# Up projection of a routed expert layer: stationary operand changed from activations to weights, with the loop unrolled by two and its addresses made in fours

## The reference

```python
def _moe2_ref(x, w_gate, w_local, w1, w2):      # x (4, 576, 512), w1 (8, 512, 1024), w2 (8, 1024, 512)
    ...
            prev_e = e
            ls = logits[b, s] - logits[b, s].max()
            p = np.exp(ls)
            p /= p.sum() + 1e-09
            h = np.maximum(x[b, s] @ w1[e], 0.0)
            out[b, s] = p[e] * (h @ w2[e])
```

## Time and profile before

| | |
|---|---|
| time, median of three runs | 987.25 us (985.24 to 988.3) |
| time of the profiled execution | 985.19 us |
| its span (first to last recorded instruction) | 983.4 us |
| PE busy | 923.3 us, 94% of the span |
| share of PE in the chain that ended last | 85% |
| experts' part of the span | from about 673 us to the end |

### The profile page before, as it was taken

How to read it: one execution, slowest core, us unless ns; L and a number is a source line. 1 busy time by engine, 2 the same in 40 slices (tenths; PEclk the granted TensorE clock), 3 DMA queues, 4 the chain that set the end, 5 groups by cost and what they waited for, 6 DMA issues and landing times.

```text
span 983.4 us, 20128 instructions
## 1 busy us (share of the span) xinstructions
PE 923.3 (94%) x7739; PEld 584.8 (59%) x7740; DVE 457.1 (46%) x843; ACT 357.5 (36%) x475; POOL 284.2 (29%) x298
## 2 busy tenths in 40 slices
PE   5899998999999999999999999928999999999996
PEld 3566666456676767677767677614555555555552
DVE  4788887464523333333333343758973773000000
ACT  3677776353211212122121112012444444444442
POOL 2467766400111102020201000002443444333331
PEclk9999999899999999999999999968999999999998
DMA  8245542525201010110101102514763672111100
GB/s 284 82 149 160 165 141 64 162 84 160 65 23 44 22 43 29 35 43 21 43 21 43 43 0 74 171 36 122 252 202 124 220 223 80 43 42 49 50 13 1
DMA packets 55340, 89.21 MB, mean 91 GB/s; under 512 B 7140, under 2 KB 26035, under 8 KB 55165
## 3 DMA queue, kind: packets, MB, share of 16 engines
q1 hardware_dynamic: 49853, 72.56, 23.7%
q0 software_dynamic: 5440, 16.00, 5.3%
HBM read 71.19 MB, written 16.55 MB: 89 GB/s over the span
## 4 chain that ended last, share of the span: by engine, by line
PE 85%; DVE 8%; DMA 3%; issue 2%; ACT 1%; SPq 1%; POOL 0%; DVEq 0%; POOLq 0%; ACTq 0%
PE psum L803 19%; PE psum L820 19%; PE psum L979 13%; PE psum L955 13%; PE psum L598 4%; PE psum L742 3%; PE psum L754 2%; PE psum L968 2%; DVE m_mem L1251 2%; DVE arena L1279 2%; PE psum L943 1%; PE psum L764 1%; PE psum L619 1%; PE psum L653 1%; PE psum L672 1%
## 5 line engine op out<-in xcount | busy, mean ns | idle before, releaser
L803 PE MATMUL psum<-m_mem,arena 128*128 (+1 forms) x1728 | 198.8, 273 | 0.3 <-DVE arena L1511 0.3
L820 PE MATMUL psum<-arena,m_mem 128*128 128x512 f16 x864 | 195.3, 379 | 0.0
L803 PEld LDWEIGHTS psum<-m_mem,arena 128*128 128x128 f16 x1728 | 168.4, 98 | 26.0 <-DVE arena L1511 0.6
L820 PEld LDWEIGHTS psum<-arena,m_mem 128*128 128x128 f16 x864 | 84.6, 98 | 90.4
L955 PE MATMUL psum<-arena,m_mem 128*128 x600 | 135.2, 382 | 0.5 <-ACT m_mem L1184 0.5
L1119 ACT ACTIVATE m_mem<-psum 128x512 f16<-128x512 f32 x72 | 43.0, 597 | 250.1 <-PE psum L803 249.1
L979 PE MATMUL psum<-arena,m_mem 128*128 x600 | 133.6, 379 | 0.0
L955 PEld LDWEIGHTS psum<-arena,m_mem 128*128 128x128 f16 x600 | 58.2, 99 | 66.6 <-issue 2.8
L1419 DVE SCALAR_TENSOR_TENSOR m_mem<-psum,m_mem 128x512 f16<-128x512 f32 x72 | 49.7, 691 | 103.4 <-ACT m_mem L1119 102.6
L979 PEld LDWEIGHTS psum<-arena,m_mem 128*128 128x128 f16 x600 | 57.7, 98 | 65.4 <-issue 0.4
L1756 POOL TENSOR_TENSOR arena<-m_mem,arena 128x1024 f16<-128x1024 f32 x9 | 18.0, 1995 | 272.2 <-ACT arena L1134 227.2
(11 more groups left out here) (220 smaller groups left out, 1156.4 us busy)
## 6 DMA issues: line engine op xcount, KB each, us to landing
dimdft_sb<-in_exp_w SPq DMA_DIRECT2D x74, 256.0 KB, 3.2
wstage<-in_exp_w SPq DMA_DIRECT2D x54, 256.0 KB, 3.2
m_mem<-in_qk SPq DMA_DIRECT2D x16, 576.0 KB, 4.5
arena<-in_v SPq DMA_DIRECT2D x32, 160.0 KB, 4.3
x_rows<-m_mem SPq DMA_DIRECT2D x16, 320.0 KB, 3.3
x_rows<-arena SPq DMA_DIRECT2D x9, 512.0 KB, 2.8
wstage<-in_mlp_w SPq DMA_DIRECT2D x16, 256.0 KB, 3.2
arena<-in_mlp_w SPq DMA_DIRECT2D x16, 256.0 KB, 2.9
```

What stands on the lines that cost most here:

```text
L803: last = nc.tensor.matmul(psum[:, 2 + k % 4, (f % 2) * 2 * P:(f % 2 + 1) * 2 * P], w1_sb[:, sp_, c, f * P:(f + 1) * P], unT[:, bass.ds(t % ...
L820: last = nc.tensor.matmul(psum[:, 6 + q, :], hT[:, k % 4, sp_, at:at + P], w2_sb[:, mp, f, :], start=f == 0 and sp_ == 0 and mp == 0, stop ...
```

## The change

`up` now takes the weights as the stationary operand and streams the activations past them. One matmul has 128x128 weights and 128 columns of tokens, so there are 8 x 4 x 3 = 96 of 128 columns in place of 24 of 512. The result is already features by tokens: `transpose_he`, `copy_heT`, `he_parts` and their semaphores go, and so do the 11 unused matmuls ahead of the last `down`. ACT's rectified parts go straight to `heT`, which now has two copies (`k % 2`), so the PE loop is unrolled by two (`turn`). `up` has a new wait for `hs_done` (banks 2 and 3 read by ACT), and `relu` new waits for `he_lo` and `blocks_done`.

```diff
+            def point(slot, places, base):
+
+                regs = [pe.alloc_register(f"weights_at{next(pointers)}") for _ in places]
+                for reg, at in zip(regs, places):
+                    pe.reg_add(reg, slot, 2 * at + base)
...
+            def pointed(at, n):
+                return slot_bytes[:, bass.ds(at, 2 * n)].bitcast(F16)
+
+            def up(k, e, slot, first):
 
                 pe.wait_ge(xeT_copied, k + 1)
                 pe.wait_ge(w_split, e * ECH + (WCH + ECH))
-                for half in range(2):
+                if not first:
+                    pe.wait_ge(hs_done, k)
+                for f in range(FE // P):
                     for c in range(DC):
-                        for sp_, mp in THREE:
-                            at = mp * EW + c * FE + half * 512
-                            last = nc.tensor.matmul(psum[:, 2 + half, :], xeT[:, sp_, c, :],
-                                                    slots[:, bass.ds(slot, 1), at:at + 512]
-                                                    .rearrange("p o n -> p (o n)"),
-                                                    start=c == 0 and sp_ == 0 and mp == 0,
-                                                    stop=c == DC - 1 and sp_ == 1)
+                        if c % 2 == 0:
+                            regs = point(slot, [wp * EW + (c + i) * FE + f * P for i in range(2) for wp in range(2)],
+                                         ARENA_AT + 2 * P - 2)
+                        for wp, mp in THREE:
+                            last = nc.tensor.matmul(psum[:, 2 + f // 4, f % 4 * P:(f % 4 + 1) * P],
+                                                    pointed(regs[wp * EW + c * FE + f * P], P), xeT[:, mp, c, :],
+                                                    start=c == 0 and wp == 0 and mp == 0,
+                                                    stop=c == DC - 1 and wp == 1)
                 last.then_inc(eh_ready, 1)
 
-            def transpose_he(k):
-
+            def down(k, turn, slot, first=False):
                 pe.wait_ge(he_lo, k + 1)
-                for i in range(2):
-                    into = psum[:, 4 + i, :].bitcast(F16)
-                    for f in range(FE // P):
-                        last = nc.tensor.transpose(into[:, f * P:(f + 1) * P], he_parts[:, i, f * P:(f + 1) * P],
-                                                   identb_sb[:, :])
-                last.then_inc(heT_ready, 1)
...
-            def experts(k, first=False, last=False, second=False):
+            def experts(k, turn, first=False, last=False, second=False):
                 e, slot = expert_of(k)
                 if not first:
                     _, last_slot = expert_of(k - 1)
-                    transpose_he(k - 1)
-                up(k, e, slot)
+                up(k, e, slot, first)
                 if not last:
                     transpose_xe(k + 1)
                 if not first:
-                    down(k - 1, last_slot, second)
+                    down(k - 1, 1 - turn, last_slot, second)
...
-            with pe.Fori(2, NBLK - 1) as k:
-                experts(k)
-            experts(NBLK - 1, last=True)
+            with pe.Fori(2, NBLK - 1, 2) as k:
+                for turn in range(2):
+                    experts(k + turn, turn)
+            experts(NBLK - 1, 0, last=True)
             _, slot = expert_of(NBLK - 1)
-            transpose_he(NBLK - 1)
-            keep_clock(2, 11)
-            down(NBLK - 1, slot)
+            down(NBLK - 1, 0, slot)
...
-            def relu(k):
+            def relu(k, first, early):
 
                 act.wait_ge(eh_ready, k + 1)
-                nc.scalar.activation(he_parts[:, 0].rearrange("p (b n) -> p b n", b=2), psum[:, 2:4, :], ACT.Relu,
+                if not first:
+                    act.wait_ge(he_lo, k)
+                if not early:
+                    act.wait_ge(blocks_done, k)
+                nc.scalar.activation(heT[:, bass.ds(k % 2, 1), 0].rearrange("p o f s -> p (o f s)"),
+                                     psum[:, 2:4, :].rearrange("p b n -> p (b n)"), ACT.Relu,
                                      scale=1.0 / WS).then_inc(he_hi, 1)
```

More of the change, by code:

```diff
@@ L21 @@
+import itertools
 import math
@@ L122, in fused_kernel @@
         x_tail = SLOT_STEP + SLOT_WORDS
+        slot_bytes = arena[:, :].bitcast(mybir.dt.uint8)
         def slot_of(e):
             return (e * 3 + 1) % NSLOT
+        ARENA_AT = 16512
         ident_sb = sb("ident_sb", [P, P], F32)
@@ L293, in fused_kernel @@
         hs = carve([FE], F32)
-        he_parts = carve([2, FE], F16)
-        heT = carve([2, FE // P, P], F16)
+        heT = carve([2, 2, FE // P, P], F16)
         xe_parts = carve([2, D], F16)
@@ L436, in fused_kernel @@
         hs_done = sem("hs_done")
-        heT_ready = sem("heT_ready")
         he_hi = sem("he_hi")
         he_lo = sem("he_lo")
-        heT_copied = sem("heT_copied")
         blocks_done = sem("blocks_done")
@@ L945, in transpose_xe @@
                 last.then_inc(xeT_ready, 1)
-            def up(k, e, slot):
+            pointers = itertools.count()
+            def point(slot, places, base):
+                regs = [pe.alloc_register(f"weights_at{next(pointers)}") for _ in places]
+                for reg, at in zip(regs, places):
+                    pe.reg_add(reg, slot, 2 * at + base)
+                return {at: pe.snap(reg, donate=True, min_val=base, max_val=base + 2 * (NSLOT * SLOT_STEP - D),
+                                    guaranteed_mod_val=0, out_of_modulus=2) - base
+                        for reg, at in zip(regs, places)}
@@ L972, in down @@
-            def down(k, slot, first=False):
-                pe.wait_ge(heT_copied, k + 1)
                 if not first:
@@ L976, in down @@
                 for f in range(FE // P):
+                    if f % 2 == 0:
+                        regs = point(slot, [mp * EW + DC * FE + (f + i) * D for i in range(2) for mp in range(2)],
+                                     ARENA_AT)
                     for sp_, mp in THREE:
[L978 to L981, removed]
+                        last = nc.tensor.matmul(psum[:, 6, :], heT[:, turn, sp_, f, :],
+                                                pointed(regs[mp * EW + DC * FE + f * D], D),
                                                 start=f == 0 and sp_ == 0 and mp == 0,
@@ L987, in expert_of @@
                 e = pe.value_load(blkexp[0:1, bass.ds(k, 1)], min_val=0, max_val=E - 1)
-                return e, pe.snap(slot_of(e))
-            def experts(k, first=False, last=False, second=False):
+                return e, pe.snap(slot_of(e) * (2 * SLOT_STEP))
+            def experts(k, turn, first=False, last=False, second=False):
                 e, slot = expert_of(k)
@@ L1004, in _ @@
             slots_second()
-            experts(0, first=True)
-            experts(1, second=True)
-            with pe.Fori(2, NBLK - 1) as k:
-                experts(k)
-            experts(NBLK - 1, last=True)
+            assert NBLK % 2 == 1
+            experts(0, 0, first=True)
+            experts(1, 1, second=True)
+            with pe.Fori(2, NBLK - 1, 2) as k:
+                for turn in range(2):
+                    experts(k + turn, turn)
+            experts(NBLK - 1, 0, last=True)
             _, slot = expert_of(NBLK - 1)
-            transpose_he(NBLK - 1)
-            keep_clock(2, 11)
-            down(NBLK - 1, slot)
+            down(NBLK - 1, 0, slot)
         @block.scalar
@@ L1185, in copy_xeT @@
                     .then_inc(xeT_copied, 1)
-            def relu(k):
+            def relu(k, first, early):
                 act.wait_ge(eh_ready, k + 1)
-                nc.scalar.activation(he_parts[:, 0].rearrange("p (b n) -> p b n", b=2), psum[:, 2:4, :], ACT.Relu,
+                if not first:
[4 more added lines that the diff above has]
+                                     psum[:, 2:4, :].rearrange("p b n -> p (b n)"), ACT.Relu,
                                      scale=1.0 / WS).then_inc(he_hi, 1)
-                nc.scalar.activation(hs.rearrange("p (b n) -> p b n", b=2), psum[:, 2:4, :], ACT.Relu, scale=1.0 / WS)\
+                nc.scalar.activation(hs, psum[:, 2:4, :].rearrange("p b n -> p (b n)"), ACT.Relu, scale=1.0 / WS)\
                     .then_inc(hs_done, 1)
[L1195 to L1200, removed]
             def weigh(k, first):
@@ L1211, in experts @@
             def experts(k, first=False, second=False, last=False):
-                if not first:
-                    copy_heT(k - 1)
-                relu(k)
+                relu(k, first, first or second)
                 if not last:
@@ L1225, in _ @@
             experts(NBLK - 1, last=True)
-            copy_heT(NBLK - 1)
             weigh(NBLK - 1, False)
@@ L1787, in he_lo_of @@
                 pool.wait_ge(hs_done, k + 1)
-                nc.gpsimd.tensor_tensor(he_parts[:, 1], hs, he_parts[:, 0], ALU.subtract).then_inc(he_lo, 1)
```

(2 more changed lines are left out.)

## The result

The changed kernel takes 970.25 us (median of four runs, 968.86 to 970.97) against 986.38 us of the kernel before, measured beside it (median of four, 985.24 to 988.3). The ratio is 0.9833, 95% interval 0.9813 to 0.9853: 1.7% faster, by 16.1 us. The forecast was 966.5, the range 962 to 979. The profiled execution took 969.82 us, its span is 968.0.

The account below looks back on a forecast made before the run. The prediction took PE's array as the bound in a steady block. Gains of 1.3 (start), 16.1 (23 blocks) and 2.0 (end), 19.4 us off 985.19, gave 965.8; it forecast 966.5 us, adjusted toward the median, range 962 to 979.

Parts of the forecast that it names:

- PE's array as the bound, and the gain per block: Steady block: array time decides; `transpose_he` saves 0.89 us, `up` at 5.37 costs 0.19 more, gaining 0.70 (0.67 to 0.73).
- The sequencer: Feeding the 96 matmuls of `up`: taken as hidden, at 59 ns a matmul against a limit of 70.
- The 46 ns of each register instruction are its own: Middle reading of PE's feeding: 51 ns a matmul, 59 with its share of one register instruction for six.
- the lower bound: Lowest estimate of feeding in `up`: matmuls at 30 ns plus a sixth of 46 ns, 38 ns each.
- the two readings: Middle and low estimates of PE's feeding in `up`, 59 and 38 ns a matmul, both under 70.
- the rival: PE's sequencer bounds `up` at up to 82 ns a matmul, making the kernel slower, 993 us; chance 0.11.
- the formula: Steady block if feeding takes 82 ns: 3.8 + 96 x 0.082 = 11.7 for 10.5, minus 0.70, plus 0.5 us.
- The lead: PE's queue holds some 17 matmuls, so feeding `up` starts 3.8 us into the 5.18 us of `down`.
- The array's pace for such a pair: In `up`, a 128x128 weight load and 128-column matmul take 55.6 to 56.2 ns; rival of more, 0.04.
- POOL's round: Rival: scatter landing 1.3 us late stretches POOL's 10.2 us round to 11.5, costing 0.5 in 23 blocks, 978 us; chance 0.06.
- The start: First blocks: `up(1)` waits only for ACT's L1184; gain 1.3 us if the clock falls again, 3.1 if it holds.
- The end: After the last blocks: 3.27 us of transposes and unused matmuls go, 1.3 of waiting comes bare; gain 2.0 us.

Follow-up runs that it names:

- addr_each: The changed kernel, but `up` makes weight addresses with one register instruction ahead of each one or two matmuls instead of one ahead of six; 1004.47 us.
- order_of_three: The changed kernel with each chunk's three products ordered high x high, low x high, high x low, so the stationary operand changes every matmul; 970.24 us in one run.

## Why the prediction was right

- **PE's array as the bound, and the gain per block.** Right. 0.66 us a block against 0.70; putting the transposes back returned 21.2 us. The term that was mis-sized is `up`, "I take 5.37": it measured 5.41, a hundredth over the upper end of 5.40, and that is 0.9 us in 23 blocks. The other order of the products gives 5.36.
- **The sequencer.** The conclusion was right, the reading that carried it was not. "The 46 ns of each register instruction are its own", so 51 ns a matmul and 59 with its share, is wrong: nearly all of the time between two register instructions (the hand-over, as the expectations call what goes beyond the recorded 46) goes with the register instruction, and the matmuls add little. The changed kernel shows it where the queue is empty, at the start of `up(0)` (source views of 675.55 to 676.1 and of 675.5 to 675.96 us):

```profile
L954 PEldq FUSED_REGOPS  x4: 42/58/60, 675.6 to 676.0; - x4
...
L974 PE MATMUL psum<-m_mem,arena x5: 217/220/227, 675.7 to 675.9; 128*128 128x128 f16 x5
```

  The four register instructions start within 0.4 us, and in the order 18 matmuls stand between them; the array began five by 675.9. So six are fed in some 0.13 us, 22 ns each, where 70 was the limit. That is under even the 38 that the prediction called the lower bound. So there was luck in it: the two readings on which it took the feeding as hidden fell under 70 with a wrong division of the time. The trace of before holds the right one: in the stretch of the earlier trace rows, twelve of the 13 gaps are 124 or 125 ns long, though one matmul stands in some and two in others. The view that the prediction read gives only the first and the last start. With one instruction for each 1.5 matmuls instead, the rival came true at 1004 us; the formula, which gave plus 0.5 us a block against before at 82 ns, was mild: 0.68 was measured. The lead was larger than worked out: in a steady block feeding began 3.4 us after the start of `down` (737.18 in the chain) where the prediction had 3.8, and paused at 741.0, 1.4 us before the array began `up` at 742.36, as a full queue would make it (source view of 738 to 742.2 us):

```profile
L954 PEldq FUSED_REGOPS  x4: 42/55/113, 740.6 to 741.0; - x4
```

- **The array's pace for such a pair.** Right, 56.4 ns against 55.6 to 56.2. The rule of the Trainium skill ("TensorE: Matmul & The Clock Gate", "Back-to-back issue gap") of about 81 ns for a sustained stream of loads and matmuls of 128 columns does not hold in this kernel: 96 in a row took 5.41 us.
- **POOL's round, the loop's body, ACT's new waits.** In the changed kernel's profile no sign of them in a steady block, as forecast. But POOL's round is close: in five of the other profiles PE waited 0.3 to 0.9 us for gathered rows in one early block. The prediction had its mechanism right (late landings) and priced it as 0.5 us in each of 23 blocks; the runs show it once.
- **The start.** 1.3 us forecast, 0.5 measured. The idle time (2.97 against 3.1), the fall of the clock and the start of `up(1)`, 9.0 us after `up(0)`, were as worked out. Missing was what comes behind: the gather for block 2 waits on POOL behind `he_lo` of block 0, and landed 0.5 us after PE was ready for it; the rest of the 0.8 is in the matmuls behind that wait, whose pipeline starts afresh (8 transposes take 0.62 us in the chain in place of 0.45).
- **The end.** 2.0 us forecast, 2.0 measured, with 1.2 us of waiting for 1.3.
- **The level.** The forecast of 966.5 was made from one execution of before at the low end of its runs. Between the profiled executions 15.4 us were won where 19.4 was worked out: 2.2 us lie ahead of `up(0)` and are not the change's, 0.9 in the blocks, 0.8 at the start. Counted from `up(0)`, 17.6 of the 19.4 came.

## What to carry to other kernels

When an operand is turned round to save a transpose, the array's time hardly moves (24 x 216 ns became 96 x 56 ns), but the sequencer has a quarter of the time for each matmul, here 56 ns in place of 216. Count its register instructions before anything else: here one for 1.5 short matmuls makes the kernel 1.8% slower than before and one for six makes it 1.7% faster, and one run with one for three is as fast. Where a phase starts with an empty pipeline, follow every queue for a block or two: shortening one wait there is worth only the distance to the next. And when the bound gets shorter, see what runs close beside it: here POOL's scatter and gather, with a round of 10.2 us in a block of 11.04, broke through in single blocks.

## What the runs showed of the hardware

- A register instruction of 37 to 60 ns between matmuls takes some 0.12 to 0.14 us of PE's sequencer, hand-over included, and the matmuls between two of them, one to six, add little or nothing: 0.123 us and 0.128 (`addr_each`) with one or two, about 0.12 with three, about 0.13 with six.
- A load of 128x128 weights at a register's address and its matmul of 128 columns follow each other at 56.4 ns, at a granted clock of 1.00, for 96 in a row; another order of the high and low parts is worth 0.5 ns of it.
- PE's queue held some 17 pairs of a load and a matmul, an estimate from the earlier trace rows.
- After 3.0 us without a matmul the granted clock was 0.50 for some 3.3 us; with 12 unused matmuls in that time `up(1)` ran at 1.00 and took 1.6 us less.
- The landing of an indirect DMA varies by a microsecond and more between executions: POOL waited 5.71 us for the first scatter in `order_of_three` and 3.68 us in the changed kernel.
